# Plain fp32 products in place of three of rounded halves, in the experts and the dense layers of an attention, mixture-of-experts and dense chain

## The reference

```
# 1 a recurrence with complex decay a (scaled to a magnitude of at most 0.999)
S_re, S_im = decay(a, S_re, S_im);  S_re += k_t v_t^T;  y_t = q_t S_re
# 2 one expert of 8 for each token, F = 1024
logits = x @ w_gate + modality_bias[modality_id]
e = argmax(logits);  g = softmax(logits)[e]
x = g * (relu(x @ w1[e]) @ w2[e])                # 384 -> 1024 -> 384
# 3 dense layers
out = (((x @ w1) * (x @ w2)) @ w3) @ w_out       # 384 -> 1024 -> 1024 -> 384
```

## Time and profile before

| | |
|---|---|
| median of 3 runs | 948.1 us (945.27 to 949.22) |
| the profiled execution, its own time | 949.64 us |
| its span, first to last instruction | 947.9 us |
| mean granted TensorE clock | 0.959 |
| busy: TensorE, VectorE, ScalarE, GpSimd | 798.0 (84%), 510.3 (54%), 344.2 (36%), 128.1 us (14%) |
| instructions on TensorE | 4598 matmul records, 4598 weight loads |
| moved by DMA | 102.95 MB |

### The profile page before, as it was taken

How to read it: one execution, slowest core, us unless ns; L and a number is a source line. 1 busy time by engine, 2 the same in 40 slices (tenths; PEclk the granted TensorE clock), 3 DMA queues, 4 the chain that set the end, 5 groups by cost and what they waited for, 6 DMA issues and landing times.

```text
span 947.9 us, 11977 instructions
## 1 busy us (share of the span) xinstructions
PE 798.0 (84%) x4598; PEld 663.3 (70%) x4598; DVE 510.3 (54%) x980; ACT 344.2 (36%) x684; POOL 128.1 (14%) x127
## 2 busy tenths in 40 slices
PE   0039800699999998999999999999999999999995
PEld 0025400388888888778888888878989888888885
DVE  4999999999898855835445445452111121202010
ACT  6921201355545335345245335342222222213120
POOL 0201100000000322200000000002223232323231
PEclk9999955799999998999999999999999999999998
DMA  9981121557666675163433342233000000000000
GB/s 382 378 274 53 59 75 27 142 142 189 173 175 173 174 196 199 52 200 105 132 120 111 104 146 88 67 78 126 25 9 17 17 9 26 9 26 1 34 0 34
DMA packets 49014, 102.95 MB, mean 109 GB/s; under 512 B 12080, under 2 KB 31792, under 8 KB 46640
## 3 DMA queue, kind: packets, MB, share of 16 engines
q1 hardware_dynamic: 43312, 83.11, 28.5%
q0 software_dynamic: 5632, 18.94, 5.7%
HBM read 64.06 MB, written 18.95 MB: 88 GB/s over the span
## 4 chain that ended last, share of the span: by engine, by line
PE 69%; DVE 19%; DMA 3%; SPq 3%; ACT 3%; issue 2%; POOL 0%; DVEq 0%
PE moe_bank L515 18%; PE moe_bank L517 18%; PE moe_bank L516 18%; PE bank L1291 4%; DVE rows L1002 3%; DVE rows L1003 3%; PE bank L1325 2%; DVE gates L1005 2%; PE bank L1341 2%; PE bank L1257 2%; DVE gates L978 2%; DVE gates L1006 2%; SPq L670 1%; DMA gates<-a_im 1%; PE bank L1345 1%
## 5 line engine op out<-in xcount | busy, mean ns | idle before, releaser
L1835 DVE TENSOR_TENSOR u_sb<-x_in,moe_bank 128x512 f32<-128x512 f32 x48 | 33.0, 688 | 229.3 <-PE moe_bank L517 229.3
L1692 POOL TENSOR_TENSOR hid_lo<-u_sb,hid_hi 128x512 fp32r<-128x512 f32 x48 | 62.4, 1300 | 387.8 <-ACT hid_hi L1741 387.8
L517 PE MATMUL moe_bank<-xT_hi,w_lo 128*128 128x512 f32 x288 | 114.1, 396 | 0.0
L515 PE MATMUL moe_bank<-xT_hi,w_hi 128*128 128x512 f32 x288 | 113.7, 395 | 0.0
L516 PE MATMUL moe_bank<-xT_lo,w_hi 128*128 128x512 f32 x288 | 113.3, 394 | 0.0
L1270 PE MATMUL bank<-early_w_out,early_w3T 128*128 128x384 f32 x128 | 45.4, 511 | 66.0 <-DMA early_w_out<-w_out 62.6
L1270 PEld LDWEIGHTS bank<-early_w_out,early_w3T 128*128 128x128 f32 x128 | 24.8, 199 | 85.9 <-issue 64.7
L1756 ACT COPY x_in<-moe_bank 128x512 f32<-128x512 f32 x48 | 28.2, 587 | 149.8 <-PE moe_bank L517 149.8
L515 PE MATMUL moe_bank<-hid_hi,w_hi 128*128 128x512 f32 x168 | 68.0, 405 | 3.9 <-DVE hid_lo L510 2.0
L517 PE MATMUL moe_bank<-hid_hi,w_lo 128*128 128x512 f32 x168 | 67.1, 400 | 0.0
L516 PE MATMUL moe_bank<-hid_lo,w_hi 128*128 128x512 f32 x168 | 67.1, 400 | 0.0
(11 more groups left out here) (196 smaller groups left out, 1698.6 us busy)
## 6 DMA issues: line engine op xcount, KB each, us to landing
stage<-w SPq DMA_DIRECT2D x12, 1536.0 KB, 7.9
ks<-mags SPq DMA_DIRECT2D x48, 144.0 KB, 2.8
x_sorted<-early_zero POOLq DMA_DIRECT2D x8, 772.0 KB, 20.8
qs<-gates SPq DMA_DIRECT2D x40, 146.2 KB
x_in<-x_sorted SPq DMA_DIRECT2D x28, 193.0 KB, 3.7
gates<-a_re SPq DMA_DIRECT2D x4, 1170.0 KB, 12.3
gates<-a_im SPq DMA_DIRECT2D x4, 1170.0 KB, 14.6
spare<-k SPq DMA_DIRECT2D x4, 1152.0 KB, 5.5
```

Source lines behind the costliest of these rows:

```text
L515: nc.tensor.matmul(out, l_hi, r_hi, start=first, stop=False)
L517: return nc.tensor.matmul(out, l_lo, r_hi, start=False, stop=last)
L1692: nc.gpsimd.tensor_tensor(hid_lo[:, f], u_sb[:, f % 2], hid_hi[:, f].bitcast(F32), ALU.subtract).then_inc(u_lo_ready, 1)
L1835: nc.vector.tensor_tensor(u_sb[:, f % 2], a_sb[:, f % 2], bank_b[f % 2][:, :], ALU.mult).then_inc(u_ready, 1)
```

## The change

Experts and dense layers take one plain fp32 matmul where they took three of halves. The copies and subtractions that made the halves go, in all three parts. Each expert weight has two buffers (even and odd steps), and w1 and w2 of step j are loaded while earlier steps run. The dense weights have buffers of their own and are loaded in steps 2, 3 and 4. The product of w3 and w_out is stored as it is. VectorE scales the tokens in all steps (ScalarE did from step 1 on). The first two output blocks of step 0 are issued in attention, behind its hidden layer. In step 1 TensorE turns the tokens behind output(0, 2), not ahead of it. TensorE's steps past 5 are nested, and the last output stands inside them.

```diff
-def split_matmul(nc, out, l_hi, l_lo, r_hi, r_lo, first, last):
-    nc.tensor.matmul(out, l_hi, r_hi, start=first, stop=False)
-    nc.tensor.matmul(out, l_hi, r_lo, start=False, stop=False)
-    return nc.tensor.matmul(out, l_lo, r_hi, start=False, stop=last)
+def relu_hidden(nc, act, L, W, bank, j, f):
+    act.wait_ge(W.hid_psum, j * L.hid.shape[1] + (f + 1))
+    nc.scalar.activation(L.hid[:, f], bank, ACT.Relu).then_inc(W.hid_ready, 1)
 def hidden(nc, pe, L, W, banks, j, f):
...
     if f >= 2:
-        pe.wait_ge(W.hid_lo_ready, j * KF + f - 1)
-    pe.wait_ge(W.w1_lo_ready, j * KF + f + 1)
+        pe.wait_ge(W.hid_ready, j * KF + f - 1)
     for k in range(KD):
         if f == 0:
-            pe.wait_ge(W.xT_lo_ready, j * KD + k + 1)
-        mm = split_matmul(nc, banks[f % 2][:, :], L.w1_hi[:, k, cols], L.w1_lo[:, k, cols], L.xT_hi[:, k], L.xT_lo[:, k],
-                          k == 0, k == KD - 1)
+            pe.wait_ge(W.xT_ready, j * KD + k + 1)
+        mm = nc.tensor.matmul(banks[f % 2][:, :], L.w1[j % 2][:, k, cols], L.xT[:, k], start=(k == 0), stop=(k == KD - 1))
     mm.then_inc(W.hid_psum, 1)
+def output(nc, pe, L, W, bank, w2, at_hid, d):
...
+    for k in range(KF):
+        if d == 0:
+            pe.wait_ge(W.hid_ready, at_hid + (k + 1))
+        mm = nc.tensor.matmul(bank[:, :], w2[:, k, cols], L.hid[:, k], start=(k == 0), stop=(k == KF - 1))
+    mm.then_inc(W.out_psum, 1)
@@ attention, ScalarE
-                    if slot == 7:
-                        act.wait_ge(W.w1_first, HU * DMA)
-                        act.wait_ge(qt_ready, 2 * B - 1)
-                        for i in range(NU):
-                            act.wait_ge(ks_in[i], B * (DMA * n_ks))
-                    for f in EARLY_W1_HI.get(slot, ()):
-                        split_w1_hi(nc, L, L.stage1, f, W.w1_hi_ready)
@@ attention, TensorE
+            pe.wait_ge(W.w1_first, HU * DMA)
             for f in range(KF):
                 hidden(nc, pe, L, W, bank_scores, 0, f)
...
+            pe.wait_ge(W.w2_first, HU * DMA)
+            pe.wait_ge(R.rank_read, B + 1)
+            for d in range(2):
+                output(nc, pe, L, W, W.first_out[d], L.w2[0], 0, d)
@@ experts, SP
+            def load_w1(j, e):
+                if j >= 2:
+                    sp.wait_ge(W.hid_psum, (j - 1) * KF)
+                sp.dma_start(L.w1[j % 2][:, :, :], ...)
+            def load_w2(j, e):
+                if j >= 2:
+                    sp.wait_ge(out_psum, (j - 1) * KD)
+                sp.dma_start(L.w2[j % 2][:, :, :], ...)
             def step(j):
+                if j > 1:
+                    load_w1(j, e)
                 sp.wait_ge(order_kept, j * DMA)
                 sp.wait_ge(W.xT_psum, j * KD)
                 load_x(sp, L, io, W, row)
-                sp.wait_ge(w1_lo_ready, j * KF)
-                sp.dma_start(stage1[:, :, :], ...)
+                if j == 1:
+                    load_w1(j, e)
+                load_w2(j, e)
                 keep_order(sp, L, io, W, j, bass.ds(at, BLOCK))
-                sp.wait_ge(w2_lo_ready, j * KF)
-                sp.dma_start(stage2[:, :, :], ...)
+                if j == 2: ... mid_w1    # j == 3: mid_w2, j == 4: last_w
@@ experts, TensorE
+            def after(j):
+                if j < NB - 1:
+                    step(j + 1)
+                    after(j + 1)
+                elif j < NS - 1:
+                    run = pe.value_load(table[0:1, L.RUN + j + 1:L.RUN + j + 2], min_val=0, max_val=1)
+                    with pe.If(run == 0):
+                        for d in range(KD):
+                            out_of(j, d)
+                    with pe.If(run != 0):
+                        step(j + 1)
+                        after(j + 1)
...
-                        mm = split_matmul(nc, bank_a[f % 2][:, :], w1_hi[:, k, cols], w1_lo[:, k, cols], xT_hi[:, k], xT_lo[:, k],
-                                          k == 0, k == KD - 1)
+                        mm = nc.tensor.matmul(bank_a[f % 2][:, :], L.mid_w1[:, k, cols], x2T[:, k, at],
+                                              start=(k == 0), stop=(k == KD - 1))
...
-                        mm = split_matmul(nc, bank_end[q % 2][:, 0:DM], hid_hi[:, k, rows], hid_lo[:, k, rows],
-                                          w2_hi[:, k], w2_lo[:, k], k == 0, k == KF - 1)
+                        mm = nc.tensor.matmul(bank_end[q % 2][:, 0:DM], hid[:, k, rows], L.last_w[:, k],
+                                              start=(k == 0), stop=(k == KF - 1))
```

More of the change, by code:

```diff
@@ L1203, in vector @@
                     V.read_rank(RANKS_AFTER[g - 1], rank, RANKS_AFTER[g - 1] == B - 3)
-                between(b, slot)
                 if g and last < NCH - 1:
@@ L1545, in vector @@
                 V.again()
-                for stale in (L.hid_hi, L.hid_lo, L.w2_hi, L.w2_lo):
-                    V.done(nc.vector.memset(stale[:, :, :].bitcast(F32), 0.0))
+                for stale in (L.hid, L.w2[0]):
+                    V.done(nc.vector.memset(stale[:, :, :], 0.0))
                 V.table_blocks()
@@ L1701, in scatter @@
                         in_=out_sb[:, t % 2, q], in_offset=None).then_inc(out_stored[t % 2], DMA)
-            pool.wait_ge(ids_ready, 1)
-            for t in range(NB):
-                rests(t)
-                scatter(t)
             for i in range(2):
@@ L1843, in output @@
                 if j:
                     pe.wait_ge(x2T_kept, (j - 1) * KD + d + 1)
[L1845 removed]
                     if d == 0:
[L1847 to L1851 removed]
+                        pe.wait_ge(w2_in[j % 2], loads(j))
@@ L1853, in step @@
+                output(nc, pe, L, W, bank_out[d], L.w2[j % 2], j * KF, d)
             def step(j):
                 if j > 1:
-                    output(j - 1, 0)
-                    output(j - 1, 1)
-                turn_x(nc, pe, L, W, bank_xT, j)
-                output(j - 1, 2)
+                    out_of(j - 1, 0)
+                    out_of(j - 1, 1)
+                    turn_x(nc, pe, L, W, bank_xT, j)
+                    out_of(j - 1, 2)
+                else:
+                    out_of(0, 2)
+                    turn_x(nc, pe, L, W, bank_xT, 1)
@@ L1859, in step @@
+                pe.wait_ge(w1_in[j % 2], loads(j))
                 for f in range(KF):
                     hidden(nc, pe, L, W, bank_hid, j, f)
-            output(0, 0)
-            output(0, 1)
-            pe.wait_ge(R.table_ready, 1)
-            last = total(pe, L.NM1, 1, 1)
-            each_step(pe, step)
-            for d in range(KD):
-                cols = slice(d * P, (d + 1) * P)
-                pe.wait_ge(x2T_kept, last * KD)
-                for k in range(KF):
-                    if d == 0:
-                        pe.wait_ge(hid_lo_ready, last * KF + (k + 1))
-                        pe.wait_ge(w2_lo_ready, last * KF + (k + 1))
-                    mm = split_matmul(nc, bank_out[d][:, :], w2_hi[:, k, cols], w2_lo[:, k, cols], hid_hi[:, k], hid_lo[:, k],
-                                      k == 0, k == KF - 1)
-                mm.then_inc(out_psum, 1)
@@ L1878, in tensor @@
-            for t in range(NB):
-                pe.wait_ge(x2T_lo_ready, t * KD + KD)
+            def after(j):
[5 more added lines that the diff above has]
+                    with pe.If(run == 0):
+                        for d in range(KD):
+                            out_of(j, d)
+                    with pe.If(run != 0):
+                        step(j + 1)
+                        after(j + 1)
+                else:
+                    for d in range(KD):
+                        out_of(j, d)
@@ L1880, in tensor @@
+            pe.wait_ge(R.table_ready, 1)
+            first_kept, all_kept = total(pe, L.NM3, KD, 1), total(pe, L.N3, KD)
+            after(0)
+            for t in range(NB):
+                pe.wait_ge(x2T_kept, all_kept if t else first_kept)
+                at = slice(t * BLOCK, (t + 1) * BLOCK)
+                if t == 0:
+                    pe.wait_ge(mid_w1_in, DMA)
+                    pe.wait_ge(mid_w2_in, DMA)
+                    pe.wait_ge(last_w_in, DMA)
                 for f in range(KF):
```

350 lines of the change are left out of this document (89 added, 261 removed).

## The result

The changed kernel takes 1063.32 us (median of 4 runs, 1062.78 to 1064.10) against 948.66 us of the kernel before in the same session (945.27 to 951.76): ratio 1.121, 95% interval 1.117 to 1.125. It is 12% slower. The forecast of 1070 us (1058 to 1090) held it, 6.7 us too high.

The account below looks back on a forecast made before the run. TensorE's stream of products was taken to bound the kernel's second half. Span 947.9 + 126.1 (products) - 5.1 (attention) + 1.4 (stalls) = 1070.3 us, forecast as 1070 us, range 1058 to 1090.

Parts of the forecast that it names:

- The products: Experts and dense layers: a plain product costs 0.858 us against 0.694 (512 columns), 0.645 against 0.521 (384); 126.1 us more.
- Four passes: Rival for experts and dense layers: a plain product costs four records at the rounded pace, 178.0 us more, 1122 us; chance 0.06.
- The stalls: TensorE's idles and following half clock in the kernel's second half: 8.4 us before, 9.8 after, so +1.4 us.
- At the table: Behind outputs 0 and 1 of step 0: TensorE's jump past the recurrence block now comes bare, 2.0 + 1.6 us.
- xT copy in step 1: Expert step 1: ScalarE's first copy of the turned tokens is no longer covered by output(0, 2), 0.8 us.
- Jump over the output block: Between expert steps 5 and 6: nesting adds one jump over the block of 24 products, 1.8 us (0 to 3.6).
- Jump out of the steps: End of the expert steps: TensorE's jump stays, now behind the last output, 3.6 us.
- Attention: Attention's last batch, slot 7: ScalarE no longer waits for the expert's weights, so TensorE's chunks shorten; gain 5.1 us.
- the early product: Product of w3T by w_out: TensorE ends at least 5.2 us earlier but then waits for VectorE's mags; zero gain.
- the loads: Expert and dense weight loads: 7.9 us to landing, issued a whole step (41.2 us of products) ahead; zero effect.
- Two records at the rounded pace: Rival for experts and dense layers: plain products cost 0.463 and 0.347 us, kernel takes 767 us; chance 0.04.
- a wait per step: Rival for expert steps 2 to 6: weights or x land late, 3.6 us each, 18 us, 1088 us; chance 0.10.

Follow-up runs that it names:

- turn_first: Changed kernel with TensorE's turning of the tokens in step 1 put back ahead of output(0, 2): 1060.02 us.
- scalar_waits: Changed kernel with ScalarE's wait for the first expert's w1 put back in slot 7 of attention's last batch, without the copies behind it: 1063.93 us.
- single_buffers: Changed kernel with one buffer each for w1 and w2, loaded later, and the dense weights loaded behind the last step: 1063.25 us.
- flat_after: Changed kernel with TensorE's steps not nested and the last output behind the jump out of the steps, with constants for step 6: 1063.09 us.
- late_w1_hi: Kernel before with ScalarE's wait and the first expert's w1_hi copies one slot later, VectorE's w1_lo too: 946.38 us, ratio 1.0009.
- nested_before: Kernel before with TensorE's steps nested and the last output ahead of the jump, as in the change: 944.99 us, ratio 0.9981.
- dense_plain: Kernel before with plain fp32 products for mid_w1 and mid_w2 only (288 products), all splits still run: 997.96 us.
- two_of_three: Kernel before with the third matmul of each rounded triple left out, all splits kept: 786.15 us.
- late_and_nested: Kernel before with w1_hi copies one slot later and TensorE's steps nested: 944.51 us, ratio 0.9975.

## Why the prediction was right, point by point

**The products: right.** Forecast 0.858 and 0.645 us a product, 1.24 times three rounded ones. Measured 2 x 0.4291 = 0.858 in the experts, 61.8 us a dense tile (forecast 61.8), and 20.64 us for 64 records of 384 columns (721.83 to the next tile at 742.47), 0.3225 each. After: 1248 x 0.4292 + 384 x 0.3225 = 659.5 us (forecast 659.2). The price came whole from two other places of the kernel before; it held for other buffers and other weights. Before was a little dearer than put: its hidden products in the experts stand 0.700 us apart (611.80 to 617.40 for eight), not 0.694, about 1 us over 168 of them. So the growth was near 125 us.

**Four passes.** The Trainium skill ("FP8 and Floating Point Precision", TensorE Precision Notes) has true FP32 at four passes. It gives no price. Taken as four rounded records that would be 4/3 of the triples, +177.7 us; the runs disagree with that reading, at 1.24 and about +125. A plain product shows as two records; how passes lie in them, no run shows.

**The stalls: mis-sized.** The forecast held 9.8 us; 3.0 came. This is the step that failed, and nearly all of the error.
- At the table: 2.0 + 1.6 forecast, 1.13 and no half clock measured.
- xT copy in step 1: 0.8 forecast, 1.89 measured. The order was read rightly (turn_first confirms it). What the term left out is ScalarE's table load of 1.28 us, which the move of scale_x, costed at nothing, put ahead of that copy. It also left out the half clock behind the wait, 1.7 us, which this execution was spared and two others (scalar_waits, single_buffers) were not.
- Jump over the output block, 1.8 forecast: nothing.
- Jump out of the steps, 3.6 forecast: nothing, and nothing even without the nesting (flat_after). The price was taken from the kernel before, where shorter products stand in front of the jump and table values behind it; which of the two matters is open.

**Attention: right in place, weak in what it rests on.** Forecast 5.1 us, measured 6.1: the rest is VectorE's routing, for which TensorE waited 0.9 us and no longer does. That the subtractions' going is the reason fits late_w1_hi, where they come later and the wait is 1.42 us. But the 5.1 us belong to the profiled execution, and the comparison of spans uses that same one, so that the term came out is luck in its size. In three others the same code loses under 1 us; from slot 7 to hidden(0) nested_before takes 22.82 us and the changed kernel 21.18, so 1.6 us is nearer to what the change gives there. The kernel before ranges from 942.73 to 952.19 us in one session, the changed one from 1062.78 to 1064.10. The profiles show three parts of that: the landing of w1, that of qs (dense_plain), and half clock that follows an idle of some 2 us in one execution and not in the next. Whether they are all is open.

**Costed at nothing, and nothing:** the splits under TensorE's stream (but see two_of_three for how thin that cover was), the early product (TensorE waits 70.6 us for mags in place of 56.6, hidden as said), the loads (single_buffers). Costed at nothing and not nothing: scale_x on VectorE, by the table load above.

**The sum against the span.** Forecast 1070.3, measured 1061.0, 9.3 less: stalls 6.8 (too high by 2.5, 1.8 and 3.6, too low by 1.1), attention 1.0, the hidden products 1.0, and 0.5 unexplained.

**The rivals.** Two records at the rounded pace fell by the distance of the records; two_of_three shows that at such a pace the change would have been a gain: 786 us, with more waits for the splits than before in it. Four passes fell by the same row, and a wait per step by TensorE's waits.

## What to carry to other kernels

Count what TensorE spends on a product by the distance between starts, not by the number of instructions or their mean duration: here one instruction for three was 24% dearer. Look for the price of a new operation in other places of the old trace; two lines outside these stages gave the sum of the products within 0.1%. Where work moves off an engine, look at what that engine does first without it: here a table load of 1.28 us moved to a copy that TensorE waits for. And do not take a stall of some 3 us in one profiled execution as the kernel's: look whether its releaser is a load that lands at different times, or a jump that the work in front may cover.

## What the runs showed of the hardware

- A plain fp32 product is two records with two weight loads, 0.4291 us each at 512 columns and 0.3225 at 384, in attention's prologue, in the experts and in the dense stage. A rounded record takes 0.2314 and 0.1735.
- A releaser in a wait can be false even when it ended 0.12 us ahead: "DVE w_lo 1.9" is gone when only TensorE's code is nested. The way out of the steps shows 3.3, 1.9, 2.1 and 0 us, as the work in front of it (and the form of the waits behind it) changes.
- The same idle is followed by half clock in one execution and not in another. Behind the wait at the table: yes after 1.95, 1.99 and 2.21 us (before, nested_before, late_and_nested), no after 1.76 and 2.34 (late_w1_hi, dense_plain). Behind the way out of the steps: yes after 1.94 and 2.13 (before, dense_plain), no after 1.99 (late_w1_hi). In the changed kernel, behind 1.89 us each time: no in after and flat_after, yes in scalar_waits and single_buffers. It costs 1.5 to 1.7 us. Neither the length alone nor the kind of product ahead decides; what does is open.
- ScalarE's table load took 1.28 us wherever it stands; it moved from L491 (411.11) to L454 (424.77) when its first operation there changed.
- The wait for w1 ranges from 1.02 to 2.67 us in executions with the same attention code, and a late load costs more than its lateness: 1.54 us more of wait than in nested_before became 1.53 us more idle of TensorE, but 2.9 us more in the chunk of slot 7, since half clock began in it, and 1.5 us more in the next.
